# Attention, routed experts and SwiGLU on one core: TensorE's wait for the gate rows put at their first use, and the first expert's weights split by GpSimd alone in the last attention pair

## What is computed

```python
scores = scale * np.matmul(q_pool, k.transpose(0, 1, 3, 2))     # 4 batches x 8 heads, 576 queries, 1152 keys
attn = softmax(scores); x = np.matmul(attn, v)                  # x becomes 2304 rows of 512
logits = x @ w_gate; e_idx = np.argmax(logits, axis=1)          # 8 experts, one for each row
gate_w = softmax(logits)[e_idx]
eom = 1.0 / (1.0 + np.exp(-(x @ w_output_gate)))
for e in range(8):
    mask = e_idx == e
    out[mask] = gate_w[mask] * eom[mask, e] * (np.maximum(x[mask] @ w1[e], 0.0) @ w2[e])
g = out @ m_gate; result = (g * sigmoid(g) * (out @ m_val)) @ m_out
```

## Time and profile before

| | |
|---|---|
| Runs | 1468.29, 1472.66 and 1474.95 us, median 1472.66 |
| The profiled execution | 1463.9 us, of it 1462.1 us of span |
| PE busy | 1355.9 us of the span (93%) |
| DVE, ACT, POOL busy | 862.8, 625.0 and 373.6 us |
| Mean granted clock of PE | 0.965 of full speed |
| Attention, routing, experts, SwiGLU | to about 617 us, to 651, to 991, to the end |

### The profile page before, as it was taken

How to read it: one execution, slowest core, us unless ns; L and a number is a source line. 1 busy time by engine, 2 the same in 40 slices (tenths; PEclk the granted TensorE clock), 3 DMA queues, 4 the chain that set the end, 5 groups by cost and what they waited for, 6 DMA issues and landing times. The chain is left out here.

```text
span 1462.1 us, 24513 instructions
## 1 busy us (share of the span) xinstructions
PE 1355.9 (93%) x7653; PEld 1196.8 (82%) x7653; DVE 862.8 (59%) x1622; ACT 625.0 (43%) x1527; POOL 373.6 (26%) x303
## 2 busy tenths in 40 slices
PE   3699999999999999729978999998999999999998
PEld 2588888888888888617867888878999999999997
DVE  2589999999999998684433444445632323232222
ACT  2478888888888887421234001004411111111111
POOL 2212222222222221677779105022101010200000
PEclk7799999999999999959989999999999999999999
DMA  7646665555555555248557213015400000000000
GB/s 165 140 108 138 136 136 129 125 126 131 125 125 125 125 125 134 85 148 245 181 184 231 88 47 105 22 44 164 125 29 15 30 15 31 15 9 14 0 22 22
DMA packets 125023, 144.91 MB, mean 99 GB/s; under 512 B 48352, under 2 KB 90848, under 8 KB 122912
## 3 DMA queue, kind: packets, MB, share of 16 engines
q1 hardware_dynamic: 109872, 103.37, 28.9%
q10 hardware_dynamic: 11648, 29.36, 6.3%
q0 software_dynamic: 3440, 11.27, 2.7%
HBM read 84.48 MB, written 19.66 MB: 71 GB/s over the span
## 5 line engine op out<-in xcount | busy, mean ns | idle before, releaser
L585 ACT ACTIVATE p_hl<-ps_t 128x512 fp32r<-128x512 f32 (+1 forms) x336 | 196.1, 586 | 93.5 <-PE ps_t L759 90.7
L709 DVE TENSOR_TENSOR p_hl<-ps_t,p_hl 128x512 fp32r<-128x512 f32 (+1 forms) x336 | 217.3, 667 | 28.2 <-ACT p_hl L585 23.6
L759 PE MATMUL ps_t<-ident,probs 128*128 128x128 f32 x1296 | 197.5, 274 | 12.7 <-DMA gate_rows<-in_moe_w_output_gate 12.1
L833 PE MATMUL ps_o<-p_hl,v_hl 128*128 128x512 f32 x576 | 205.8, 438 | 1.2 <-DVE kept_rows L659 1.2
L759 PEld LDWEIGHTS ps_t<-ident,probs 128*128 128x128 f32 x1296 | 161.0, 141 | 39.3 <-issue 12.8
L601 ACT ACTIVATE probs<-ps_s_late,neg_max 128x384 f32<-128x384 f32 x288 | 165.1, 578 | 29.2 <-DVE neg_max L652 27.2
L1661 ACT ACTIVATE silu<-ps_g 128x384 f32<-128x384 f32 x72 | 35.4, 492 | 315.4 <-PE ps_g L1767 315.4
L867 PE MATMUL ps_s_late<-kq_t 128*128 128x384 f32 x640 | 159.7, 361 | 8.4 <-ACT probs L601 7.6
L1714 DVE TENSOR_TENSOR silu<-ps_g,silu 128x384 f32<-128x384 f32 x72 | 40.1, 557 | 211.3 <-ACT silu L1661 211.3
L1083 POOL TENSOR_TENSOR w_parts<-raw_w,w_parts 128x1024 fp32r<-128x1024 f32 x56 | 132.1, 2399 | 97.8 <-ACT w_parts L1156 97.8
L1156 ACT ACTIVATE w_parts<-raw_w 128x1024 fp32r<-128x1024 f32 x56 | 58.3, 1057 | 216.3 <-POOL w_parts L1083 95.0
(11 more groups left out here) (198 smaller groups left out, 2840.8 us busy)
## 6 DMA issues: line engine op xcount, KB each, us to landing
raw_w<-in_moe_w ACTq DMA_DIRECT2D x56, 512.0 KB, 4.2
kq_t<-kept_rows SPq DMA_DIRECT2D x32, 608.0 KB, 6.3
kq_t<-kept_rows SPq DMA_DIRECT2D x32, 320.0 KB, 7.1
raw_k<-in_k SPq DMA_DIRECT2D x32, 288.0 KB, 5.6
raw_v<-in_v SPq DMA_DIRECT2D x16, 576.0 KB, 4.9
kq_t<-kept_rows SPq DMA_DIRECT2D x32, 288.0 KB, 6.6
raw_q<-in_q SPq DMA_DIRECT2D x32, 256.0 KB, 4.0
y_by_slot<-x_out SPq DMA_DIRECT2D x25, 256.0 KB, 2.0
```

Of the source, the lines that this page charges most:

```text
L585: nc.scalar.activation(p_hi[prob_ring(kind, m)][:, 0:w], T[ring(kind, j)][:, 0:w], ACT.Copy).then_inc(hi_ready, 1)
L709: nc.vector.tensor_tensor(p_lo[n][:, 0:w], t[:, 0:w], p_hi[n][:, 0:w].bitcast(F32), ALU.subtract).then_inc(t_free, 1)
L759: last = nc.tensor.transpose(dst[:, n * P:(n + 1) * P], src, ident[:, :])
L833: last = nc.tensor.matmul(O[:, :], v_hl[v_par][:, c * P:(c + 1) * P], part[:, :], start=(i == 0 and n == 0), stop=(i == CH - 1 and n == 1))
```

## The change

PE's two waits move from the end of the first pair to the first `x` step of every later pair. POOL's constants for routing are made before the last pair's splitting. POOL makes the first parts of w1[0] when the scores of the pair before last are done, their rests at the old place, and all of w2[0] (first parts and rests) when the last scores are done. SP puts three of the four loads of w2[0] ahead of the store of a pair's x, and one behind. In routing ACT no longer makes first parts of w2[0], and POOL's rests of expert 1 all stand behind the gathers into `kept` and ahead of the seven late ones.

```diff
 # SP, last pairs
-                store(LAST - 1, 0, "last")
-                for j in range(RAW):
+                def load_down(j):
                     sp.wait_ge(shared.w_ready[0], j + 1)
                     sp.dma_start(shared.early_raw[j]..., w2[0]...[j]).then_inc(shared.early_loaded[j], 16)
+                for j in range(RAW - 1):
+                    load_down(j)
+                store(LAST - 1, 0, "last")
+                load_down(RAW - 1)
                 store(LAST, 1, "tail")
 # POOL, last pair
-                pool.wait_ge(pv_done, upto(LAST, "last", is_prob, ("c", 2)))
-                for j in range(RAW):
-                    pool.wait_ge(shared.early_loaded[j], 16)
...
-                    if j == 1:
-                        sum_gates(LAST, LAST % 2, "last", late)
 # POOL, after the constants
+                pool.wait_ge(s_ready, MAXIMA * LAST)
+                for j in range(RAW):
+                    pool.wait_ge(shared.early_loaded[j], 16)
+                    first_of(0, j)
+                pool.wait_ge(pv_done, upto(LAST, "last", is_prob, ("c", 2)))
+                for j in range(RAW):
+                    second_of(0, j)
+                sum_gates(LAST, LAST % 2, "last", late)
+                pool.wait_ge(s_ready, MAXIMA * PAIRS)
+                for j in range(RAW):
+                    pool.wait_ge(shared.early_loaded[j], 32)
+                    first_of(1, j)
+                    second_of(1, j)
 # PE, step x and the end of the first pair
+                        if i == 0:
+                            pe.wait_ge(gate_rows_ready, 4)
+                            pe.wait_ge(gates_loaded, 16 * 8)
...
-                    if kind == "first":
-                        pe.wait_ge(gate_rows_ready, 4)
-                        pe.wait_ge(gates_loaded, 16 * 8)
 # POOL, routing
-                residues(0, 0, range(W1P, PIECES))
-                residues(1, 1, range(W1P))
...
                 for i in range(KEPT):
                     gather(shared.kept[:, i * D:(i + 1) * D], FIRST + i, kept_gathered)
+                residues(1, 1)
                 for i in range(LATE):
                     gather(xs_late[:, i * D:(i + 1) * D], TILES - LATE + i, last_gathered)
-                residues(1, 1, range(W1P, PIECES))
 # ACT, routing
-                first_parts(0, 0, ring_wait=False, pieces=range(W1P, PIECES))
...
-                first_parts(1, 1, ring_wait=False, pieces=range(W1P))
-                act.wait_ge(w_ready[1], W2P)
-                first_parts(1, 1, ring_wait=False, pieces=range(W1P, PIECES))
+                first_parts(1, 1, ring_wait=False)
```

More of the change, by code:

```diff
@@ L557, in _, with first_of, second_of @@
                 pool.wait_ge(gates_chain, 4)
-                nc.gpsimd.tensor_scalar(w[upper, :], w[upper, :], float(D), None, ALU.subtract)
+                nc.gpsimd.tensor_scalar(w[upper, :], w[upper, :], float(D), None, ALU.subtract).then_inc(gates_chain, 1)
+                pool.wait_ge(gates_chain, 5)
+                def first_of(n, j):
+                    at = j * PIECE
+                    z = zeros[:, :].rearrange("p (o d) -> p o d", o=1).broadcast_to([P, PIECE // P, P])
+                    nc.gpsimd.tensor_tensor(
+                        w_sb[n][:, at:at + PIECE].rearrange("p (o d) -> p o d", d=P),
+                        shared.early_raw[j][:, :].rearrange("p (o d) -> p o d", d=P), z, ALU.add
+                    ).then_inc(shared.w_hi_done, 1)
+                def second_of(n, j):
+                    at = j * PIECE
+                    pool.wait_ge(shared.w_hi_done, RAW * n + j + 1)
+                    nc.gpsimd.tensor_tensor(w_sb[n][:, WCOLS + at:WCOLS + at + PIECE], shared.early_raw[j][:, :],
+                                            w_sb[n][:, at:at + PIECE].bitcast(F32), ALU.subtract
+                                            ).then_inc(shared.w_ready[n], 1)
+                pool.wait_ge(s_ready, MAXIMA * LAST)
[11 more added lines that the diff above has]
+                    second_of(1, j)
             @block.scalar
@@ L1141, in first_parts @@
                                                              min_val=1, max_val=TILES + 1))
-                    early = isinstance(e, int) and e == 0
                     for j in pieces:
@@ L1150, in first_parts @@
                             act.wait_ge(down_done, down_limit)
-                        if early:
-                            act.wait_ge(shared.early_loaded[j % RAW], 32)
-                        else:
-                            act.wait_ge(raw_loaded[j % RAW], 16 * ((PIECES // RAW) * (e - 1) + j // RAW + 1))
-                        nc.scalar.activation(w_part(n, parity, 0, at, PIECE), source(e, j), ACT.Copy
+                        act.wait_ge(raw_loaded[j % RAW], 16 * ((PIECES // RAW) * (e - 1) + j // RAW + 1))
+                        nc.scalar.activation(w_part(n, parity, 0, at, PIECE), raw[j % RAW][:, :], ACT.Copy
                                              ).then_inc(w_hi_done, 1)
                         ahead = j + RAW - 1
-                        if early or (isinstance(e, int) and e == 1 and j == 0):
+                        if isinstance(e, int) and e == 1 and j == 0:
                             continue
```

12 lines of the change are left out of this document (1 added, 11 removed).

## The result

The changed kernel takes 1451.99 us (median of 4 runs, 1449.61 to 1455.41) against 1470.47 us for the kernel before on the same chip: a ratio of 0.9888 [0.9864, 0.9911]. Six more runs of it gave 0.9878 [0.9852, 0.9904]. Its profiled execution took 1450.36 us, with a span of 1448.6, 13.5 us less than before. The predicted ratio was 0.987.

What follows compares the result with a forecast made beforehand. The prediction took PE to bound the kernel, so only its waits could be won: 14.3 - 1.8 + 14.5 - 6.4 - 2.0 = 18.6 us, taken from the median 1472.66 to give 1454.1 us, range 1445 to 1463.

Steps and rivals of the forecast that it cites:

- Case A: The forecast itself, all terms as worked out: 1454.1 us; chance 0.66.
- new waits of PE: Two moved gate-row waits in each later pair, put at 0, at most 1 us in all.
- part 1: Gate rows, first pair to pair 1: the 12.1 us wait and 2.2 us of slow clock go, gain 14.3 us.
- Neither waits: In pair 1, neither pair 2's query sums (2.6 us early) nor the gate rows would hold PE up.
- rival D: The gate wait turns up elsewhere, at g of pair 1, and 14.3 us are lost: 1468.4; chance 0.07.
- part 2: Routing: DVE's small instructions no longer wait for POOL's current one, gain 14.5 us.
- part 3: Experts: up(1) waits 6.4 us for POOL's rests and loses 2.0 us of clock; expert 2's splits start at 697.5.
- part 4: Last pair and tail: L677 waits for POOL's instruction, cost 1.8 us (0 to 2.4); L680 does not wait.
- The sum: All terms together: 18.6 us off the profiled execution, carried over to the median.
- B: Rival: up(1) hardly waits, up to 8.4 us more gained, 1445.7; chance 0.09.
- C: Rival: routing gives nothing in the end, the wait at up(1) eating all 14.5 us, 1460.2; chance 0.15.
- E: Rival: the chain of weights falls behind at expert 2's splits; 35 us late gives 1481.7; chance 0.03.

Runs made afterwards that it cites:

- e1: The kernel before with only PE's two waits for the gate rows moved to step x of later pairs; ratio 0.9920 to the kernel before.
- e6: The changed kernel with eight POOL additions of 128x1024 put beside DVE's chain in routing; routing took 33.76 us against 23.54.
- e7: The changed kernel with eight POOL memsets of 128x2304, which read nothing, put beside DVE's chain in routing; routing took 34.16 us against 23.54.
- e4: The changed kernel with POOL's rests of expert 1's w1 made after three kept tiles' gathers, ahead of the other six; ratio 0.9865 to the kernel before.
- e9: e4 with DVE's coefficient chain moved ahead of the parts of the first tiles' rows; ratio 0.9880 to the kernel before.
- e12: The changed kernel with the edits of e3 and e9, a small first zeros DMA, and tile 0's store ahead of the late tiles' save; 1438.24 us, ratio 0.9791.
- e3: The changed kernel with the tail's nine row sums put into unused columns of a PSUM bank; ratio 0.9839 to the kernel before.

## Why the prediction was right, point by point

Predicted 1454.1 (1445 to 1463), a ratio of 0.987; measured 1451.99, 0.9888. Case A is what happened: every mechanism that it names is in the trace. That three terms also agree to a tenth of a us is in part luck, as the means over several traces show (mean of before's code against mean of the changed code):

| Term (us) | predicted | this pair of traces | means of the traces |
|---|---|---|---|
| gate rows, to pair 1's last c product | -14.3 | -14.26 | -12.2 |
| new waits of PE | 0 to +1 | +1.09 | +0.9 |
| tail | +1.8 | +5.50 | +3.4 |
| routing | -14.5 | -14.54 | -14.5 |
| up(1), wait and clock | +8.4 | +8.42 | +6.9 |

- **The gate rows** (part 1, gain 14.3): 14.26 in the trace, 13.3 if counted from the end of the first pair; 12.2 in the mean of eight traces, and e1 alone is worth 11.8 by its runs. The changed kernel's trace was one of the two best of the eight. The sentence that failed is "Neither waits": the two transfers it named were in time, but a third one, the zeros behind the gate rows in SP's queue, was not looked at. DVE waited 1 to 3 us for it. That is rival D at another step and for much less than 14 us. The new waits of PE were put at 0, "at most 1 in all"; the runs give 0.9.
- **Routing** (part 2, 14.5): 14.54. POOL was to leave over 2 us to spare before attention's end; it left 7.6, of which 5.5 are the longer tail itself. The reason, DVE held up by POOL's current instruction, is shown by e6 and e7, which bring back 10 of the 14.5 with POOL alone.
- **up(1)** (part 3, a wait of 6.4 and 2.0 of clock): the stretch behind up(0) grew by 8.42. With POOL's order unchanged it takes 92.93 to 93.92 us in seven traces, but 84.73, 86.01 and 88.95 with before's code, so that the growth is 6.9 in the mean: at up(1) before loses clock too in some executions, which part 3 didn't count. e4, e9 and e12 show that it is POOL's order that sets it, and that POOL's order isn't the only thing behind it: two more dependences lay just below the surface. The start of expert 2's splits is mis-added in part 3: 674.6 and 24.0 make 698.6, not 697.5. Measured, the splits came 53.1 us behind the start of up(0) (685.44 - 632.31), where part 3 has 57.5 (697.5 - 640.0). There was slack on this chain, so neither moved the time.
- **The tail** (part 4, "Cost 1.8 (0 to 2.4)"): this is the term that was mis-sized. It cost 5.5 in this pair of traces and 3.4 in the mean. L677 waited 1.6 us and the reciprocal didn't, as worked out. But the step took a wait of DVE for its own length. PE was already pausing 1.4 us at this place, the two add to 2.9, and PE's clock fell for the rest of the block, in all eight traces with that pause against three of the six with the short one. Part 3 had priced the clock behind a wait and part 4 hadn't. e3 takes the wait away, and in its trace the 5.5 with it. The 2.4 of the range was no bound at all.
- **The sum** (18.6): in the profile 13.5, in the means of the traces 15.5, in the runs 16.5 and about 18. Between profiles it is the tail's 3.7, the 1.1 of the extra waits and the 0.3 at the end that are missing. That the runs gave more than the profiles comes with before's quick profiled execution; the prediction took its distance of 8.8 us to the median over to the changed kernel, whose own profiled execution is only 1.6 under its median. The two misses have opposite signs, and the closeness of 1454.1 to 1451.99 owes something to that.
- **Rivals.** B (no wait at up(1)) fell: 6.53. C (nothing from routing) fell: routing kept its 14.5 and the wait at up(1) took 6.5 of them. E (the chain of weights late) fell: the waits before up(8) and up(9) are 7.83 and 3.96, against 7.83 and 4.62.

## What to carry to other kernels

When a wait is taken away, list every transfer in the queues that it had covered, not only those that the next steps name: here the zeros, the coefficient product and tile 0's store each came up in turn, and only with the last of them out of the way did the early gathers pay. A delay of DVE before a point where PE already pauses is priced as the sum of the two pauses, plus what the clock may cost in the stretch behind it, as a range. Before one trace is held against another, take a second one of the same kernel: here the same code took 6 us longer at two places of one execution than of another. Before an instruction of DVE is put beside POOL, look where its operands lie: the same nine columns in PSUM didn't wait.

## What the runs showed of the hardware that was not expected

- One DVE product with two SBUF inputs was held up through four subtractions of POOL in a row, 9.18 us (e4), while in the kernel before each such instruction waited for one of them, 2.06 to 2.27. What makes the difference isn't settled. The Trainium skill (SBUF — State Buffer, "SBUF: two separate sides") gives the lock for one whole instruction; the wait in e4 was longer than that.
- A wait of PE whose semaphore is long there costs about 0.03 us, an estimate from 28 of them: the middle of attention takes 490.69 to 490.95 us in three traces without them and 491.19 to 491.98 in eleven with them.
- With the same instructions and the same pauses, PE's clock falls in some executions and not in others: behind a pause of 1.4 us it stayed at 1.00 to the end of attention in before (a tail of 31.44 us) and fell to 0.50 in e1 (33.55). Behind a pause of 2.9 us it fell in all eight traces, at once or within 3 us, and the tail took 34.88 to 36.94.
